# Expert list in seven pieces, last chunk in two pieces, shared first loads: one change to a fused DFT, mixture-of-experts and channel-mix kernel

## The reference, cut to what matters

```python
X = np.fft.fft(np.fft.fft(x, axis=1), axis=2).real   # x: (4, 3072, 256)
# experts: N = 12288 rows, D = 256, E = 8, F = 1024
idx = argmax(norm(x) @ norm(expert_emb).T / tau); gate = softmax(...)[idx]
out[idx == e] = gate * (relu(x[idx == e] @ w1[e]) @ w2[e])
# channel mix over tokens, x_prev = the token before (zeros ahead of token 0)
xk = mu_k*x + (1-mu_k)*x_prev;  xr = mu_r*x + (1-mu_r)*x_prev
out = sigmoid(xr @ w_r) * (relu(xk @ w_k)**2 @ w_v)
```

## Time and profile before

| | us |
|---|---|
| median of 3 runs (lowest, highest) | 1460.26 (1455.94, 1460.77) |
| the profiled execution, its own time | 1464.79 |
| its span, first to last instruction | 1462.6 |
| PE busy | 1410.7 (96%) |
| DVE busy | 1088.7 (74%) |
| ACT busy | 872.3 (60%) |
| mean granted TensorE clock | 0.983 of 2.4 GHz |
| DFT stage, to the last L671 matmul | 0 to 200 |
| experts | 204.4 to 851.2 |
| channel mix on PE | 866.9 to 1456.2 |

### The profile page before, as it was taken

How to read it: one execution, slowest core, us unless ns; L and a number is a source line. 1 busy time by engine, 2 the same in 40 slices (tenths; PEclk the granted TensorE clock), 3 DMA queues, 4 the chain that set the end, 5 groups by cost and what they waited for, 6 DMA issues and landing times.

```text
span 1462.6 us, 27267 instructions
## 1 busy us (share of the span) xinstructions
PE 1410.7 (96%) x9048; PEld 1287.7 (88%) x9048; DVE 1088.7 (74%) x1806; ACT 872.3 (60%) x1683; POOL 248.1 (17%) x225
## 2 busy tenths in 40 slices
PE   8998889999899999999999969999999999999998
PEld 7887778999899999999999958888888888888886
DVE  5776776977577677777777748787878787878784
ACT  2564475666576666666666636565656565656563
POOL 2144426553231111111111110000000000000000
PEclk9999999999999999999999989999999999999999
DMA  8324257889776776677767521313121212121211
GB/s 245 95 82 122 105 181 224 273 281 317 253 233 198 231 216 214 223 248 230 221 209 229 189 44 30 58 30 57 29 57 29 54 33 53 33 50 36 49 23 29
DMA packets 208662, 201.49 MB, mean 138 GB/s; under 512 B 189961, under 2 KB 191863, under 8 KB 199992
## 3 DMA queue, kind: packets, MB, share of 16 engines
q1 hardware_dynamic: 198712, 175.45, 42.5%
q0 software_dynamic: 9888, 25.28, 5.2%
HBM read 160.44 MB, written 42.06 MB: 138 GB/s over the span
## 4 chain that ended last, share of the span: by engine, by line
PE 89%; DVE 3%; issue 3%; DMA 2%; SPq 1%; ACT 1%; POOL 0%; POOLq 0%; DVEq 0%; ACTq 0%
PE ps L606 80%; PE ps L633 3%; PE ps L671 3%; DMA we_raw<-w_e 1%; PE ps L658 1%; PE ps L659 1%; DVE we L1098 1%; DMA rows<-xr,pos 1%; DVE zv L1122 0%; DVE zu L1122 0%; SPq L432 0%; SPq L517 0%; DVE ht L1170 0%; PE ps L597 0%; ACT we L792 0%
## 5 line engine op out<-in xcount | busy, mean ns | idle before, releaser
L606 PE MATMUL ps<-x_split,w_split 128*128 128x512 f32 x1440 | 331.9, 390 | 12.8 <-DVE x_split L1224 12.8
L606 PE MATMUL ps<-we,ht 128*128 128x256 f32 x2640 | 329.3, 283 | 4.9 <-DVE ht L1170 4.8
L606 PE MATMUL ps<-xgt,we 128*128 128x256 f32 x2640 | 326.4, 282 | 7.9 <-DVE we L1098 4.3
L606 PEld LDWEIGHTS ps<-x_split,w_split 128*128 128x128 f32 x1440 | 271.3, 188 | 69.5 <-issue 13.0
L606 PEld LDWEIGHTS ps<-we,ht 128*128 128x128 f32 x2640 | 323.0, 190 | 6.3 <-DVE ht L1170 6.1
L606 PEld LDWEIGHTS ps<-xgt,we 128*128 128x128 f32 x2640 | 320.1, 190 | 9.3 <-issue 9.2
L1098 DVE TENSOR_TENSOR we<-we_raw,we 128x1024 fp32r<-128x1024 f32 x220 | 264.0, 1221 | 21.9 <-ACT we L792 21.0
L606 PE MATMUL ps<-k_split,w_split 128*128 128x512 f32 x1152 | 265.0, 389 | 0.0
L1170 DVE SCALAR_TENSOR_TENSOR ht<-ps,ht 128x512 fp32r<-128x512 f32 x220 | 146.3, 686 | 151.7 <-ACT ht L850 133.3
L606 PEld LDWEIGHTS ps<-k_split,w_split 128*128 128x128 f32 x1152 | 216.2, 188 | 44.9
L792 ACT CAST we<-we_raw 128x1024 fp32r<-128x1024 f32 x220 | 224.8, 1046 | 7.6 <-DMA we_raw<-w_e 7.6
(11 more groups left out here) (130 smaller groups left out, 1095.0 us busy)
## 6 DMA issues: line engine op xcount, KB each, us to landing
we_raw<-w_e SPq DMA_DIRECT2D x55, 2048.0 KB
xg<-rows SPq DMA_DIRECT2D x220, 64.0 KB
xm<-moe SPq DMA_DIRECT2D x96, 128.0 KB, 2.8
out<-yc SPq DMA_DIRECT2D x96, 128.0 KB, 2.7
xin<-x SPq DMA_DIRECT2D x15, 768.0 KB, 7.7
rows<-tailc SPq DMA_DIRECT2D x9, 258.0 KB
moe<-yo,meta POOLq DMA_INDIRECT x110
rows<-xr,pos POOLq DMA_INDIRECT x96
```

The costliest lines, as they stand in the source:

```text
L606: ins = mm(o, a(i), b_(k), start=first_ and n == 0, stop=last_ and n == 2)
```

## The change

- The chains of tiny ops for the expert list are cut into seven functions (`tier_a`, `tier_a2`, `tier_b`, `tier_take`, `tier_c`, `tier_d`, `tier_e`), called at steps 4 to 10 of batch 2, and for the second list during tiles 4 to 9. The ops are the same.
- `place(b-1)` moves from behind chunk 5 to the end of step 1. `gate(b-1)` moves from behind chunk 7 to step 0, where DVE has nothing else, so its place in DVE's order is the same.
- The last chunk's copy and its sums are done in two pieces (`d_parts`): the slots of frequencies 0 to 2 (24 of 96 columns in each of four groups), then the other 72. `feature_dft(0)` waits for the first piece (`z_first`) and for chunk 6; `sequence_dft(0)` waits for the rest.
- `d_bank` is turned by one, so that chunks 6 and 7 lie in banks 2, 3 and 4, 5. With it the first three chunks of a batch wait for other things: chunk 0 for DVE's `ab` of k2 = 11, chunk 1 for all `eo` copies, chunk 2 for ACT's `ab` of k2 = 12.
- Channel mix: the four stripes of tile 0 are issued two by SP and two by ACT; its four tiny transfers are replaced by a memset. PE starts a tile when half c = 0 of the k input is split (`c_x0`) and waits for `c_xs` before c = 1.

```diff
-            return 2 * (c % 3)
+            return 2 * ((c + 1) % 3)
+        def d_parts(c):
+            cut = 2 * K_FIRST * J          # K_FIRST = 3, J = 4
+            return ((0, cut), (cut, KP)) if c == NC - 1 else ((0, KP),)
...
-            load_c(0, 0)
+            for a in range(2):
+                load_stripe(sp, 0, 0, a)
             load_c(1, 1)
...
-                    if c < 2:
-                        pe.wait_ge(ab_ready[c], ab_count(NK - 1 - c, b - 1))
-                    elif c == 2:
+                    if c in (0, 2):
+                        k2 = NK - 2 if c == 0 else NK - 1
+                        pe.wait_ge(ab_ready[k2 % 2], ab_count(k2, b - 1))
+                    elif c == 1:
                         pe.wait_ge(eo_ready, b * NK + PRIME)
...
                     if k2 == 0:
-                        for n in range(2):
-                            pe.wait_ge(z_done[n], (b + 1) * (NC // 2))
+                        pe.wait_ge(z_done[0], (b + 1) * (NC // 2))
+                        pe.wait_ge(z_first, b + 1)
...                                                   # sequence_dft
+                    if k2 == 0:
+                        pe.wait_ge(z_done[1], (b + 1) * (NC // 2))
...
-                pe.wait_ge(c_xs, t * 2 + 1)
+                pe.wait_ge(c_x0, t + 1)
...
+                        if f == 0 and c == 1:
+                            pe.wait_ge(c_xs, t * 2 + 1)
...                                                   # ACT
-                    copy(d0[c % 2], ps[:, d_bank(c), 0:GC * KP]).then_inc(d0_ready, 1)
+                    for lo, hi in d_parts(c):
+                        copy(d0[c % 2]...[:, :, lo:hi], ps[...][:, :, lo:hi]).then_inc(d0_ready, 1)
...
+            for n in range(2):
+                act.wait_ge(scattered[n], 16 * HB * len(range(n, NB, 2)))
+            for n in range(2):
+                act.wait_ge(s_split[n], len(C_SPLIT_AT))
+            for a in range(2, P // Q):
+                load_stripe(act, 0, 0, a)
...                                                   # DVE, chunk phase
-                    dve.wait_ge(d0_ready, b * NC + c + 1)
-                    for z, op in ((zu, ALU.add), (zv, ALU.subtract)):
+                    for n, (lo, hi) in enumerate(d_parts(c)):
+                        dve.wait_ge(d0_ready, b * (NC + 1) + c + n + 1)
+                        for z, op in ((zu, ALU.add), (zv, ALU.subtract)):
...
+                        if hi < KP:
+                            last.then_inc(z_first, 1)
-                    if b and c == 5:
-                        place(b - 1)
-                    if b and c == 7:
-                        gate(b - 1)
...                                                   # DVE, step phase
+                    if b and st == 0:
+                        gate(b - 1)
+                    if b and st == 1:
+                        place(b - 1)
+                    if b == 2 and st == 4:
+                        tier_a(False)             # 3 ops
+                    if b == 2 and st == 5:
+                        tier_a2(False)            # 5 ops
                     if b == 2 and st == 6:
-                        tier_a(False)
+                        tier_b(False)             # 4 ops
+                    if b == 2 and st == 7:
+                        tier_take()               # 3 ops
                     if b == 2 and st == 8:
-                        tier_b(False)
+                        tier_c(False)             # 2 ops
+                    if b == 2 and st == 9:
+                        tier_d(False)             # 4 ops
                     if b == 2 and st == 10:
-                        tier_c(False)
+                        tier_e(False)             # 2 ops
...                                                   # DVE, channel mix
+            dve.wait_ge(w_low, NB * WP)
+            v.memset(xc[0][:, :, 0:1], 0.0).then_inc(c_zero, 1)
+            dve.wait_ge(c_zero, 1)
...
+                        if m_ == 0 and c == 0:
+                            last.then_inc(c_x0, 1)
```

More of the change, by code:

```diff
@@ L73 @@
 PRIME = 1
+K_FIRST = 3
 WORK = 49400
@@ L305, in fft_moe_channel_mix @@
         z_done = [sem(f"z_done{n}") for n in range(2)]
+        z_first = sem("z_first")
         d0_ready = sem("d0_ready")
@@ L349, in fft_moe_channel_mix @@
         c_omm = sem("c_omm")
+        c_zero = sem("c_zero")
         c_xv = sem("c_xv")
@@ L359, in fft_moe_channel_mix @@
         c_xs = sem("c_xs")
+        c_x0 = sem("c_x0")
         c_r = sem("c_r")
@@ L365, in fft_moe_channel_mix, with tile_in, load_stripe @@
         c_out = [sem(f"c_out{n}") for n in range(2)]
+        moe_flat = moe.rearrange("b r c -> (b r) c")
         block = ctx.enter_context(nc.Block())
-        TILE_IN, TILE_OUT = 16 * (2 * P // Q), 16 * (P // Q)
+        FIRST_IN, TILE_IN = 16 * (P // Q), 16 * (2 * P // Q)
+        TILE_OUT = 16 * (P // Q)
+        stripes = [(slice(a * Q, (a + 1) * Q), slice(a * DC * Q, (a + 1) * DC * Q)) for a in range(P // Q)]
+        def tile_in(t, s):
+            return t // 2 * TILE_IN + (FIRST_IN if s == 0 else TILE_IN)
+        def load_stripe(eng, t, s, a):
+            lanes, cols = stripes[a]
+            eng.dma_start(xm[s][lanes].rearrange("i t c f -> i t (c f)"),
+                          moe_flat[bass.ds(t * TC + t // (S // TC) + 1, TC), cols].rearrange("(t i) f -> i t f", i=Q)
+                          ).then_inc(c_in[s], 16)
         def wait(eng, s, n):
@@ L530, in load_c @@
                 r0 = t * TC + t // (S // TC)
[L531 to L535, removed]
+                for a in range(P // Q):
+                    load_stripe(sp, t, s, a)
                 for lanes, cols in stripes:
@@ L818, in _ @@
                         act.wait_ge(z_done[c % 2], b * (NC // 2) + c // 2)
-                    copy(d0[c % 2], ps[:, d_bank(c), 0:GC * KP]).then_inc(d0_ready, 1)
+                    for lo, hi in d_parts(c):
+                        copy(d0[c % 2].rearrange("p (g k) -> p g k", g=GC)[:, :, lo:hi],
+                             ps[:, d_bank(c), 0:GC * KP].rearrange("p (g k) -> p g k", g=GC)[:, :, lo:hi]
+                             ).then_inc(d0_ready, 1)
                     if b and c == 2:
@@ L1042, in tier_a, with tier_a2 @@
                 t_link(copy(full[:], quot8[:]))
+            def tier_a2(last):
                 t_link(v.tensor_tensor(avail[:], full[:], used[:], ALU.subtract))
@@ L1057, in tier_b, with tier_take @@
                     a, z = z, a
[L1058 to L1061, removed]
+            def tier_take():
+                t_link(v.tensor_scalar(take[:], sums[1][:, 4:4 + E], -1.0, float(TIERS[0][1]), ALU.mult, ALU.add))
+                t_link(v.scalar_tensor_tensor(take[:], take[:], 0.0, avail[:], ALU.max, ALU.min))
+                t_link(v.tensor_tensor(used[:], used[:], take[:], ALU.add))
             def tier_c(last):
@@ L1070, in tier_c, with tier_d @@
                 t_link(v.tensor_reduce(who[:, 0:n], seg[:, 0:n, 0:E - 1], AX.X, ALU.add))
+            def tier_d(last):
+                i0, n = TIERS[last]
+                m = E if last else E - 1
                 t_link(v.tensor_tensor(segd[:, 0:n, 0:m], seg[:, 0:n, 0:m],
@@ L1076, in tier_c, with tier_e @@
                 t_link(v.tensor_scalar(where[:, 0:n], where[:, 0:n], row0[:], float(E * CAPR), ALU.add, ALU.min))
+            def tier_e(last):
+                i0, n = TIERS[last]
                 t_link(copy(expert_of[:, i0:i0 + n], who[:, 0:n]))
@@ L1200, in m_step @@
                         tier_a(True)
+                    if i == 5:
+                        tier_a2(True)
+                    if i == 6:
                         tier_b(True)
-                    if i == 5:
+                    if i == 7:
                         tier_c(True)
+                    if i == 8:
+                        tier_d(True)
+                    if i == 9:
+                        tier_e(True)
             pairs(dve, LEAD, NB, m_step)
@@ L1294, in _ @@
                     for c in range(NC):
-                        pool.wait_ge(d0_ready, b * NC + c + 1)
+                        pool.wait_ge(d0_ready, b * (NC + 1) + c + 1)
                         scatter_row()
```

8 lines of the change are left out of this document (3 added, 5 removed).

## The result

| | before | after |
|---|---|---|
| median, us | 1459.38 (4 runs) | 1442.97 (1442.83 to 1445.04, 4 runs) |
| ratio of the two | | 0.9888, 95% interval 0.9876 to 0.9901 |
| profiled execution, own time / span | 1464.79 / 1462.6 | 1442.9 / 1440.9 |
| mean granted TensorE clock | 0.983 | 0.989 |

That the time came out within 1.0 us of it is in part luck: the median of before is now 0.9 us lower than the one that the forecast was counted from, and the saving itself is 1.9 us smaller. The first view is again PE's waits: engine, line, waited for, us in total, times, longest. In the changed kernel L679 is `feature_dft`, L694 `sequence_dft`, L626 the matmul of the last two stages.

A forecast was written before the change was run, and what follows sets the result against it. PE, busy 96% of the span, was the bound, losing time only in waits or at low clock. Joints 12.9, batch 0 0.1, list 3.0 and channel-mix start 2.3 summed to 18.3 us: 1442.0 from the 1460.26 median, range 1434 to 1451.

The forecast's parts named there:

- The joints: Joints of batches 1 to 3: PE's wait for the last zv falls from 3.36 to 1.1 us, 2.25 saved each.
- The op that no row of before showed: DVE's strided 96-element op on the last chunk's first piece, taken at 0.23 us, between 0.18 and 0.72.
- The clock behind the joints: Behind joints of batches 1 to 3, low-clock loss of 1.78 + 2.63 + 1.78 = 6.2 us gone; bounds 0 and 6.2.
- the clock falls anyway: Rival, chance 0.17: the clock falls behind the shorter joint waits too; 12.1 us saved, 1448.2.
- The list: Expert list in batch 2: cost falls from 4.1 to 1.1 us, 3.0 saved, between 1.5 and 4.1.
- The slack of 0.36: Steady DFT steps: each odd copy_ab has 0.36 us to spare, so an even-step piece costs its size less 0.36.
- both zeros: Chunk 1's wait for all eo copies (1.1 us of cover) and the second list in tiles 4 to 9 cost 0.
- The start of channel mix: First channel-mix tile: 1.6 us from loads and 0.68 from early c_x0, sum 2.3, between 1.2 and 2.8.
- The loads' own lower end: Channel-mix start: if tile 0's stripes wait for each other's data, last landing 861.2, 1.2 us gained.
- signs of being wrong: Low clock behind joints, 96-element op above 0.3 us, waits at sequence_dft(0) or (1), stripes landing later than 861.2.
- Batch 0: Joint of batch 0: 0.1 us gained; wait for experts_b stays near 2.7 us with its low clock.
- The stall in the first expert tiles: Rival, chance 0.05: the 3.6 us "issue" stall may grow or go, 7 us either way: 1449 or 1435.

The follow-up runs named there:

- e1: Kernel before with only the joint part: place moved, last chunk in two pieces, banks turned; list and channel-mix start as before; ratio 0.9916.
- e4: Kernel before with only place (and gate) moved, place to the end of step 1; last chunk whole, banks as before; 1450.64 us, ratio 0.9935.
- e12: Same kernel as e4, run again unchanged; 1453.33 us, ratio 0.9958.
- e8: Changed kernel with list pieces moved to odd steps 3 to 11 of batch 2, the last two to batch 3's chunks; 1441.39 us, ratio 0.9876.
- e7: Changed kernel with all four stripes of channel mix's tile 0 issued by SP, none by ACT; 1440.89 us, ratio 0.9871.
- e11: e8 with e7's edit added (all four stripes of tile 0 issued by SP); 1439.68 us, ratio 0.9858.
- e9: Kernel before with only the two-piece last chunk and turned banks; place stays behind chunk 5; 1450.38 us.
- e5: The changed kernel once more, unchanged, as reference beside the experiments; 1441.94 us, ratio 0.9874.
- e10: Changed kernel without the early c_x0 start: PE waits for both halves of the k input before each tile; ratio 0.9874.

## Why the prediction was right

**The joints.** The step was 3.36 to 1.1 us of wait, 2.25 saved in each. Measured: 1.1 to 1.2, and 6.8 us less in three. The op that no row of before showed, 96 elements with a stride, was taken at 0.23 us and follows in 0.22 (one lasts 0.31, of which 0.09 overlaps the next). `place` behind step 1 ran from 77.23 to 78.37, and DVE still idled 0.34 us ahead of its next combination, so it was covered. `copy_ab(1)` and the rest piece made nobody wait.

**The clock behind the joints.** 6.2 us were taken as lost before and as gone after. From `feature_dft(0)` to the next chunks batch 1 took 26.99 us before and 25.31 after; batch 2 took 31.92 before and 29.41 in e1, where the list stands as before and the clock doesn't fall; batch 3 took 31.57 and 29.88. That is 1.68 + 2.51 + 1.69 = 5.9 us. The rival (the clock falls anyway, 0.17) is refuted for waits of this length: behind none of the 24 waits of 1.1 to 1.2 us, in eight executions, did it fall. The reason that I gave, a limit somewhere between 1.9 and 2.8 us, was wrong: e4's clock fell behind 1.9, and in batch 0 of three executions it fell behind 1.5 and 1.8 (last section). The forecast held since none fell at 1.1. The Trainium skill (TensorE: Matmul & The Clock Gate, Part 1: The HAM clock gate) says of the warm-up that the gate runs free of the kernel, so that one kernel changes clock at different points from run to run; e4 and e12 agree, for the falls behind a wait.

**The list.** Forecast 4.1 to 1.1 us, 3.0 saved. Measured in the steps of batch 2: 29.41 with the lumps, 26.91 with the pieces, 25.31 with none in the way (batch 1 of e1 and of the changed kernel; batch 2 of e8 25.32), thus 4.1 to 1.6, 2.5 saved. `sequence_dft(5)` to `(11)` of batch 2 in the changed kernel (the rows of L694 alone; the last has `(12)` too):

```profile
128.10 1.25 PE L694 MATMUL ps<-ab,f 128*128 128x290 f32 x4
130.18 1.14 PE L694 MATMUL ps<-ab,f 128*128 128x290 f32 x4
132.79 1.25 PE L694 MATMUL ps<-ab,f 128*128 128x290 f32 x4 [0.48 <-DVE ab L798]
134.86 1.14 PE L694 MATMUL ps<-ab,f 128*128 128x290 f32 x4
137.15 1.25 PE L694 MATMUL ps<-ab,f 128*128 128x290 f32 x4 [0.15 <-DVE ab L798]
139.22 1.14 PE L694 MATMUL ps<-ab,f 128*128 128x290 f32 x4
141.32 2.23 PE L694 MATMUL ps<-ab,f 128*128 128x290 f32 x8 [0.47 <-DVE ab L798]
```

Two steady steps take 2 x 1.97 = 3.94 us. So the pieces of steps 6 and 8 shift PE by 4.69 - 3.94 = 0.75 and 4.36 - 3.94 = 0.42 where 0.57 and 0.23 were forecast. Both are 0.18 to 0.19 too small, and the starts one by one show two terms in it. The larger was not in the forecast at all: behind each late start the four matmuls take 1.25 us and not 1.14, and the next ones follow after 2.07 or 2.08 and not 1.97. That is 0.1 us for each of three late starts. e1 has the same behind its lump, with no piece of the list in the odd step that follows:

```profile
128.71 1.14 PE L693 MATMUL ps<-ab,f 128*128 128x290 f32 x4
131.83 1.25 PE L693 MATMUL ps<-ab,f 128*128 128x290 f32 x4 [0.99 <-DVE ab L797]
133.91 1.14 PE L693 MATMUL ps<-ab,f 128*128 128x290 f32 x4
```

The smaller is the slack. The start itself is late by 0.21, 0.64 and 0.32 us where the forecast has 0.21, 0.57 and 0.23: of pieces of 0.57, 0.93 and 0.59 us, 0.36, 0.29 and 0.27 were absorbed. The slack of 0.36, read from steady steps, held for the first piece and was 0.07 to 0.09 smaller for the two that follow an odd step with a piece of its own; behind e1's lumps, with free odd steps, it was 0.35 to 0.37. Why it shrinks isn't shown. Three times 0.1 and the 0.16 of slack make up the 0.5 us between 1.1 and 1.6. That PE's listed waits for `ab` add up to the forecast's 1.1 us is chance: they leave out the first late start and the longer matmuls, and count 0.47 us at the end, of which PE makes up all but 0.12.

**Banks, and the second list.** No wait at chunk 1 and none for the list in the expert tiles is listed: both zeros held.

**The start of channel mix.** Forecast 2.3 us (1.2 to 2.8), measured 1.5 over the traces: 0.9 where I took 1.6, and 0.6 where I took 0.68. The mis-sized term is the landing. I took the 2.8 us of the earlier trace rows, a median over stripes of which each came 0.48 us behind the one before; issued two at once, with those of tile 1 right behind, they took:

```profile
xm<-moe SPq DMA_DIRECT2D x6, 128.0 KB, 4.1
xm<-moe ACTq DMA_DIRECT2D x2, 128.0 KB, 3.6
```

(changed kernel, DMA issues of 830 to 845, median us to landing; the last of ACT's took 4.04). The loads' own lower end, 1.2, was not low enough. Two of the prediction's signs of being wrong came with it: DVE started 4.57 us behind the first issue, not 3.9 or less, and the last stripe landed 4.5 us behind it, where 861.2 stood for 4.2. The other signs came out as forecast, the 96-element op's 0.3 us to within 0.01. The Trainium skill's rule that was weighed against the row (DMA: Bandwidth & Descriptors, Issuing engines are not separate DMA queues) was the better guide: e7 and e11 with four stripes on SP needed 4.96 and 4.58 us from the first issue to DVE's start, and the changed kernel 4.57, so that the second issuing queue is worth 0 to 0.4 us.

**Batch 0.** Forecast 0.1 us gained, and 1.85 lost in the trace. The wait is 2.6 us as forecast. In the changed kernel's execution the clock fell ahead of the wait, in windows in which PE was busy:

```profile
22.00:24.00 2.00, 2.00 (x15) 2.00 (x15) 0.72 (x1) 0.00 (x0) 0.00 (x0) 0.72 0.73 193
24.00:26.00 2.00, 1.27 (x6) 1.03 (x5) 0.42 (x2) 0.54 (x2) 0.00 (x0) 0.50 0.07 21
```

In e9, with the same chunks, it didn't fall there or behind the wait:

```profile
24.00:26.00 2.00, 1.29 (x12) 1.12 (x11) 0.40 (x2) 0.54 (x2) 0.00 (x0) 1.00 0.16 48
26.00:28.00 2.00, 0.07 (x1) 0.10 (x1) 1.83 (x11) 0.00 (x0) 0.00 (x0) 1.00 1.12 269
28.00:30.00 2.00, 2.00 (x15) 1.89 (x16) 0.30 (x2) 0.53 (x3) 0.00 (x0) 1.00 0.93 254
```

From `feature_dft(0)` to the chunks of batch 1 it took 25.3 us in e7 and e9, and 26.8 to 28.3 in the other twelve executions, before and changed kernel among them. In seven of the fourteen the clock fell ahead of the wait, in five at it, in two not at all. e5, the changed kernel again, is one of the five: it is the execution, not the change, though why the clock may fall there under load is open.

**The sum.** 6.8 + 5.9 + 2.5 + 1.5 = 16.7 us by the traces, 16.4 by the medians, 18.3 forecast. The clock was taken 0.3 us too high, the list 0.5 and the start 0.8. The two profiled executions alone show 1.07 us for channel mix as a whole: the clock stayed at 0.50 for 3.1 us behind PE's start in the one and for 4.1 in the other, and PE started 1.5 us sooner, not the 2.3 that e10's text has. Over all traces the time from the last `yo` op to the last `yt` is 602.3 to 603.5 us (median 602.9) in the six that start as before and 600.8 to 602.3 (median 601.5) in the eight others, which bears out about 1.5. The stall in the first expert tiles (0.05) can't be judged as a rival: it was in the profiled execution of before and in none of the thirteen others, so it made the profiled execution slower and not the kernel, and the forecast from the median was right not to count on it.

## What to carry to other kernels

Price a wait of PE by its length and by the clock behind it, and bring it down to a length behind which no trace shows a fall: here 1.2 us, while from 1.5 us on it could come in one execution and stay away in the next. A late start costs more than its wait: 0.1 us here each time, which no list of waits shows. Slack read from steady steps is an upper bound where the steps before are no longer steady. Before a phase of one profiled execution enters a sum, compare that execution's own time with the median; 7 us of this one belonged to a stall that no other execution had.

## What the runs showed of the hardware

Fourteen executions were profiled. The table has each wait of PE of 0.97 us and more in their DFT stages (from 8 us on, to the last joint), and whether the clock went from 1.00 to 0.50 within the wait or the 2 us behind it:

| wait, us | where | waits | clock fell |
|---|---|---|---|
| 1.0 | first two lumps of the list | 12 | 0 |
| 1.1 to 1.2 | joints of batches 1 to 3 | 24 | 0 |
| 1.3, 1.5 | `xin`, batch 0 of e7, e5 | 2 | 1 (1.5) |
| 1.8 | `xin`, batch 0 of e10, e12 | 2 | 2 |
| 1.9 | third lump of the list | 6 | 1 (e4) |
| 2.2 to 2.4 | joints of batches 1 to 3 | 9 | 3 |
| 2.6 to 2.8 | joint of batch 0, begun at 1.00 | 7 | 5 |
| 3.3 to 3.5 | joints of batches 1 to 3 | 9 | 9 |

Seven more joints of batch 0 (2.6 to 2.8 us) began when the clock had already fallen with PE busy, so their low clock says nothing of the wait. One of the `xin` waits and the clock behind it, in e10:

```profile
11.31 9.02 PE L654 MATMUL ps<-f,xin 128*128 128x96 f32 x64 [1.83 <-DMA xin<-x]
...
12.00:14.00 2.00, 2.00 (x11) 2.00 (x11) 1.93 (x3) 0.00 (x0) 0.00 (x0) 0.50 0.96 270
```

A fall behind the wait of a joint cost 1.4 to 2.7 us, the one behind e4's lump 1.1; the three behind waits of 2.2 us cost 1.98, 1.39 and 1.64, so that with a third of them falling a wait of 2.2 to 2.4 us has an expected price of its length and about 0.6 us. I had expected a sharp limit between 1.9 and 2.8; the rows show none between 1.5 and 2.8. What sets the moment stays open: no run placed a wait of one length at a chosen moment.

The second thing is the loads. The four 128 KB stripes of tile 0 landed in 2.2 to 2.7 us each when SP issued them alone, 0.4 to 0.5 us apart (before), in 2.5 to 3.4 when SP issued tile 1's right behind them (e7), and in 2.6 to 4.0 when SP and ACT issued them together. The last of the four was there 4.1, 4.9 and 4.5 us behind the first issue: beside e7, two issuing engines saved 1.0 us of issuing and lost 0.6 of it in the landing, and in e11, with the loads of e7, the last was there after 4.5.
